# Batch 0's score products in three fp32r products for two tiles of each group of three, with the splits on ScalarE and VectorE and half of the squares' adds on GpSimd

## The reference

```python
qn = q / (norm(q, axis=1) + 1e-06)            # q, k, v: (2, 6016, 256); the norm runs over the tokens
kn = k / (norm(k, axis=1) + 1e-06)
s = kn.transpose(0, 2, 1) @ qn / tau          # (2, 256, 256): a product over 6016 tokens
a = softmax(s - s.max(-1))                    # with 1e-9 added to the sum
x = (v @ a).reshape(12032, 256)
h = x @ w_in                                  # w_in (256, 2048)
x = (h - tanh(h)) @ w_out                     # w_out (2048, 256)
out = (sigmoid(x @ w_gate) * (x @ w_val)) @ w2_out   # (256, 1536) twice, (1536, 256)
```

## Time and profile before

| what | us |
|---|---|
| median of 3 runs | 2383.25 |
| lowest and highest of them | 2382.99, 2384.51 |
| the profiled execution | 2383.25 |
| its span | 2381.5 |
| TensorE busy | 2356.5 |
| VectorE busy | 1406.4 |
| ScalarE busy | 536.5 |
| GpSimd busy | 251.2 |

### The profile page before, as it was taken

How to read it: one execution, slowest core, us unless ns; L and a number is a source line. 1 busy time by engine, 2 the same in 40 slices (tenths; PEclk the granted TensorE clock), 3 DMA queues, 4 the chain that set the end, 5 groups by cost and what they waited for, 6 DMA issues and landing times.

```text
span 2381.5 us, 29344 instructions
## 1 busy us (share of the span) xinstructions
PE 2356.5 (99%) x10410; PEld 1943.7 (82%) x10410; DVE 1406.4 (59%) x2180; ACT 536.5 (23%) x861; POOL 251.2 (11%) x130
## 2 busy tenths in 40 slices
PE   8999999999999999999999999999999999999998
PEld 7778888888888888888878888888888888888887
DVE  6856556566565565665756455555565565565553
ACT  5412122121121211212222122121221121221221
POOL 1721201202112021021310000000000000000000
PEclk9999999999999999999999999999999999999999
DMA  7400000000000000000100000000000000000000
GB/s 256 128 27 27 27 9 27 24 18 26 17 26 26 9 26 17 26 26 9 40 27 18 9 9 17 9 9 9 9 17 9 9 17 9 9 17 9 0 9 9
DMA packets 34272, 60.74 MB, mean 26 GB/s; under 512 B 3008, under 2 KB 22208, under 8 KB 34240
## 3 DMA queue, kind: packets, MB, share of 16 engines
q1 hardware_dynamic: 34240, 60.32, 7.7%
HBM read 47.99 MB, written 12.32 MB: 25 GB/s over the span
## 4 chain that ended last, share of the span: by engine, by line
PE 95%; DVE 3%; DMA 1%; issue 0%; ACT 0%; SPq 0%; POOL 0%; ACTq 0%; DVEq 0%
PE ring L236 54%; PE X L236 23%; PE O L582 17%; PE X L451 1%; DVE g_parts L913 1%; DVE g_parts L911 1%; DVE work L900 1%; PE O L236 0%; DMA v_raw<-v_t 0%; DMA qk_raw<-k 0%; POOL win_parts L386 0%; ACT work L745 0%; DVE norm L852 0%; SPq L262 0%; SPq L271 0%
## 5 line engine op out<-in xcount | busy, mean ns | idle before, releaser
L236 PE MATMUL ring<-x_parts,gv_parts 128*128 128x502 f32 x3456 | 836.8, 392 | 0.8 <-ACT x_parts L751 0.8
L745 ACT ACTIVATE work<-ring 128x502 f32<-128x502 f32 x672 | 397.1, 591 | 1680.5 <-PE ring L236 1618.7
L236 PEld LDWEIGHTS ring<-x_parts,gv_parts 128*128 128x128 f32 x3456 | 650.7, 189 | 138.5 <-issue 1.2
L236 PE MATMUL X<-g_parts,wout_parts 128*128 128x502 f32 x2304 | 579.7, 392 | 8.1 <-DVE g_parts L913 8.1
L236 PE MATMUL ring<-v_parts,weff 128*128 128x502 f32 x2304 | 585.2, 391 | 0.2 <-DVE weff L881 0.2
L236 PEld LDWEIGHTS X<-g_parts,wout_parts 128*128 128x128 f32 x2304 | 435.7, 190 | 101.3 <-DVE g_parts L913 10.9
L236 PEld LDWEIGHTS ring<-v_parts,weff 128*128 128x128 f32 x2304 | 434.2, 189 | 93.0 <-DVE work L900 2.6
L897 DVE TENSOR_TENSOR work<-work,ring 128x502 f32<-128x502 f32 x288 | 195.1, 677 | 511.8 <-PE ring L236 511.4
L582 PE MATMUL O<-p_parts,w2out_parts 128*128 128x502 f32 x1728 | 441.3, 389 | 3.3 <-DVE p_parts L911 3.2
L900 DVE TENSOR_TENSOR work<-ring,work 128x502 f32<-128x502 f32 x384 | 260.8, 679 | 266.2 <-ACT work L745 266.2
L582 PEld LDWEIGHTS O<-p_parts,w2out_parts 128*128 128x128 f32 x1728 | 324.6, 188 | 76.4 <-DVE p_parts L913 4.4
(11 more groups left out here) (71 smaller groups left out, 450.0 us busy)
## 6 DMA issues: line engine op xcount, KB each, us to landing
v_raw<-v_t SPq DMA_DIRECT2D x24, 502.0 KB, 3.6
out_t<-out_sb SPq DMA_DIRECT2D x44, 251.0 KB, 2.2
qk_raw<-q SPq DMA_DIRECT2D x24, 256.0 KB, 2.7
qk_raw<-k SPq DMA_DIRECT2D x24, 256.0 KB, 2.9
qk_raw<-q SPq DMA_DIRECT2D x15, 384.0 KB, 3.6
qk_raw<-k SPq DMA_DIRECT2D x15, 384.0 KB, 5.0
w_raw<-w_out SPq DMA_DIRECT2D x7, 512.0 KB, 3.8
w_raw<-w_in SPq DMA_DIRECT2D x4, 512.0 KB, 7.8
```

Source lines behind the costliest of these rows:

```text
L236: ins = nc.tensor.matmul(out, w[c][a], x[c][b], start=first and n == 0, stop=last and n == len(terms) - 1, skip_group_check=True)
L745: nc.scalar.activation(work[:, slot(kind, n, last), :], bank(kind, n, last), ACT.Sigmoid if kind == "p" else ACT.Tanh).then_inc(act_done, 1)
```

## The change

For groups 1 to 15 the last tile of the group stays in plain fp32. The first two tiles are split into high and low parts and multiplied as three fp32r products. Group 0 stays in fp32. The parts lie in a new tensor `qk_parts` with two slots. The splitting is shared out: VectorE copies q to its high part and subtracts for both low parts, ScalarE copies k to its high part. The sum of squares is shared out as well: VectorE adds only two of q's tiles, GpSimd adds q's third tile and k's three tiles.

```diff
+            qk_parts = sb("qk_parts", [P, 2, 2, 2, G - 1, C], F32R, a1)
...
             pool.memset(ident[:, :], 0.0).then_inc(consts_set, 1)
-            pool.memset(sq_acc[:, :, :, :], 0.0).then_inc(acc_cleared, 1)
+            pool.memset(sq_acc[:, :, :, :], 0.0).then_inc(k_acc_done, 1)
...
+            def add_squares(g, s):
+
+                pool.wait_ge(sq_done, g + 1)
+                pool.wait_ge(k_acc_done, g + 1)
+                if isinstance(g, int) and g == 0:
+                    acc, sq = sq_acc[:, 1, 0:2, :], qk_sq[:, s, 1, 0:2, :]
+                else:
+                    acc, sq = (x.rearrange("p x t c -> p (x t) c")[:, 2:2 * G, :]
+                               for x in (sq_acc[:, :, :, :], qk_sq[:, s]))
+                pool.tensor_tensor(acc, acc, sq, ALU.add).then_inc(k_acc_done, 1)
...
-            def group0(g, count, rs, u):
-
+            def group0(g, rs, s, u):
+
+                first = isinstance(g, int) and g == 0
                 pe.wait_ge(qk_loaded[rs], u * 32 + 32)
...
                 for m in range(CK):
-                    if m == norms_at:
+                    for t in ((0, 1) if first else (G - 1,)):
+                        ins = nc.tensor.matmul(X[:, m, 0:C], qk_raw[:, rs, 1, t, m * P:(m + 1) * P],
+                                               qk_raw[:, rs, 0, t, :], start=first and t == 0,
+                                               stop=first and t == 1, skip_group_check=True)
+                if not first:
+                    if isinstance(g, int) and g == GROUPS - 1:
                         norms(0)
...
+                    pe.wait_ge(qk_lo_done, g)
+                    ins = scores([qk_parts[:, s, a] for a in range(2)], G - 1, lambda m: X[:, m, 0:C], False)
                 ins.then_inc(s_done, 1)
...
                 if not (isinstance(g, int) and g < 2):
-                    act.wait_ge(acc_done, g - 1)
+                    act.wait_ge(q_acc_done, g - 1)
+                    act.wait_ge(k_acc_done, g)
                 raw = qk_raw[:, rs, :, 0:count, :]
                 nc.scalar.activation(qk_sq[:, s, :, 0:count, :], raw, ACT.Square).then_inc(sq_done, 1)
+                if not (isinstance(g, int) and g == 0):
+                    if not (isinstance(g, int) and g < 3):
+                        act.wait_ge(s_done, g - 1)
+                    nc.scalar.activation(qk_parts[:, s, HI, 1, :, :], qk_raw[:, rs, 1, 0:G - 1, :],
+                                         ACT.Copy).then_inc(k_hi_done, 1)
...
-            def group0(g, count, s):
-
-
+            def group0(g, rs, s, u):
+
+
+                first = isinstance(g, int) and g == 0
+                dve.wait_ge(qk_loaded[rs], u * 32 + 32)
+                if not first:
+                    if not (isinstance(g, int) and g < 3):
+                        dve.wait_ge(s_done, g - 1)
+                    V.tensor_copy(qk_parts[:, s, HI, 0, :, :], qk_raw[:, rs, 0, 0:G - 1, :]).then_inc(q_hi_done, 1)
                 dve.wait_ge(sq_done, g + 1)
...
-                    dve.wait_ge(acc_done, g)
-                acc = sq_acc[:, :, 0:count, :]
-                V.tensor_tensor(acc, acc, qk_sq[:, s, :, 0:count, :], ALU.add).then_inc(acc_done, 1)
+                    dve.wait_ge(q_acc_done, g)
+                acc = sq_acc[:, 0, 0:2, :]
+                V.tensor_tensor(acc, acc, qk_sq[:, s, 0, 0:2, :], ALU.add).then_inc(q_acc_done, 1)
+                if not first:
+
+                    dve.wait_ge(k_hi_done, g)
+                    dve.wait_ge(q_hi_done, g)
+                    for x in range(2):
+                        ins = V.tensor_tensor(qk_parts[:, s, LO, x, :, :], qk_raw[:, rs, x, 0:G - 1, :],
+                                              qk_parts[:, s, HI, x, :, :].bitcast(F32), ALU.subtract)
+                    ins.then_inc(qk_lo_done, 1)
```

More of the change, by code:

```diff
@@ L120, in attention_moe_kernel @@
         sq_done = sem("sq_done")
-        acc_cleared = sem("acc_cleared")
-        acc_done = sem("acc_done")
+        k_hi_done = sem("k_hi_done")
+        q_hi_done = sem("q_hi_done")
+        qk_lo_done = sem("qk_lo_done")
+        q_acc_done = sem("q_acc_done")
+        k_acc_done = sem("k_acc_done")
         s_done = sem("s_done")
@@ L380, in _ @@
                                pattern=[[-1, P]], channel_multiplier=1).then_inc(consts_set, 1)
+            def add_squares(g, s):
[7 more added lines that the diff above has]
+                pool.tensor_tensor(acc, acc, sq, ALU.add).then_inc(k_acc_done, 1)
+            for g in range(QK_SLOTS):
+                add_squares(g, g % 2)
+            with nc.Fori(0, GROUPS // QK_SLOTS - 1, engines=[ENG.Pool]) as t:
+                for s in range(QK_SLOTS):
+                    add_squares(t * QK_SLOTS + (QK_SLOTS + s), s % 2)
             def split_unit(n):
@@ L438, in scores @@
                 return ins
-            def group0(g, count, rs, u):
+            def group0(g, rs, s, u):
+                first = isinstance(g, int) and g == 0
                 pe.wait_ge(qk_loaded[rs], u * 32 + 32)
[L443 to L446, removed]
                 for m in range(CK):
-                    if m == norms_at:
-                        norms(0)
[L450 to L454, removed]
+                    for t in ((0, 1) if first else (G - 1,)):
[4 more added lines that the diff above has]
+                    if isinstance(g, int) and g == GROUPS - 1:
+                        norms(0)
+                    pe.wait_ge(qk_lo_done, g)
+                    ins = scores([qk_parts[:, s, a] for a in range(2)], G - 1, lambda m: X[:, m, 0:C], False)
                 ins.then_inc(s_done, 1)
@@ L461, in norms @@
                     pe.wait_ge(consts_set, 3)
-                    pe.wait_ge(acc_done, GROUPS)
+                    pe.wait_ge(q_acc_done, GROUPS)
                 else:
@@ L470, in norms @@
                 for n, (x, t, m) in enumerate(order):
+                    if b == 0 and n == 2 * CK:
+                        pe.wait_ge(k_acc_done, GROUPS + 1)
                     at = x * CK + m
@@ L721, in unit_hi @@
                     act.wait_ge(s_done, GROUPS)
-                    act.wait_ge(acc_done, GROUPS)
+                    act.wait_ge(q_acc_done, GROUPS)
+                    act.wait_ge(k_acc_done, GROUPS + 1)
                 if n == 2 * PIECES:
@@ L818, in _ @@
             V = nc.vector
-            def group0(g, count, s):
+            def group0(g, rs, s, u):
[5 more added lines that the diff above has]
+                    V.tensor_copy(qk_parts[:, s, HI, 0, :, :], qk_raw[:, rs, 0, 0:G - 1, :]).then_inc(q_hi_done, 1)
                 dve.wait_ge(sq_done, g + 1)
-                if isinstance(g, int) and g == 0:
-                    dve.wait_ge(acc_cleared, 1)
-                else:
-                    dve.wait_ge(acc_done, g)
-                acc = sq_acc[:, :, 0:count, :]
-                V.tensor_tensor(acc, acc, qk_sq[:, s, :, 0:count, :], ALU.add).then_inc(acc_done, 1)
+                if first:
+                    dve.wait_ge(k_acc_done, 1)
+                else:
+                    dve.wait_ge(q_acc_done, g)
[8 more added lines that the diff above has]
+                    ins.then_inc(qk_lo_done, 1)
             steps = [0]
@@ L958, in _ @@
             for g in range(QK_SLOTS):
[L959 removed]
+                group0(g, g, g % 2, 0)
             with nc.Fori(0, GROUPS // QK_SLOTS - 1, engines=[ENG.DVE]) as t:
                 for s in range(QK_SLOTS):
[L962 removed]
+                    group0(t * QK_SLOTS + (QK_SLOTS + s), s, s % 2, t + 1)
             dve.wait_ge(tau_loaded, 16)
```

6 lines of the change are left out of this document (3 added, 3 removed).

## The result

The changed kernel takes 2411.48 us (median; 2410.14 to 2412.71), the kernel before 2383.22 (2382.99 to 2384.51). The ratio is 1.0114, with a 95% interval of 1.0102 to 1.0126: 28.3 us slower. The forecast was 2417.5 us, 6 us too much; the direction was right.

What follows compares the result with a forecast made beforehand. TensorE bounds the kernel; in batch 0's score stage VectorE and GpSimd, excluding each other, would take the lead. Scaling 32.6 us later plus 1.6 us for the clock, on 2383.25, gave 2417.5 us; own range 2410 to 2423, widened to 2405 to 2425.

Steps and rivals of the forecast that it cites:

- The mechanism: In batch 0's score stage, VectorE instructions with all inputs in SBUF and GpSimd's adds run one after the other; chance 0.72.
- TensorE's saving: Score products per group: 2.29 us in place of 2.59, giving back 4.5 us only if TensorE stayed the one waited for.
- sign that was named: Trace readings expected in batch 0's score stage: group distance, scaling time, TensorE idle and GpSimd busy time, unchanged blocks.
- Rival A: Score stage: GpSimd's add runs beside VectorE's work, 2.4 us per group, 2382.4 us in all; chance 0.07.
- Rival B: Score stage: VectorE slips in cheaply between GpSimd's always-ready instructions, 3.46 us per group, 2400 us; chance 0.11.
- rival C: Score stage: TensorE at half the clock becomes the bound, some 4.9 us per group, 2423 us; chance 0.10.
- The price of a group: Score stage: GpSimd's 2.41 us plus VectorE's 2.22 us, one after the other, 4.63 us for each of 15 groups.
- The stage's end: End of batch 0's scores: last subtraction near 79.4 us, then last products and norms until the scaling at 83.7 us.
- S: Start of VectorE's scaling, the first step needing finished scores: forecast 83.7 us, before 51.12, so 32.6 us later.
- The clock: A lower granted TensorE clock, in the open only in the score stage's last matmuls: 1.6 us added.
- the tail: TensorE's work closing the score stage: twelve products, two fp32 matmuls, norms, last twelve products and draining, 6.5 us.
- Behind S: After the scaling: nothing taken; v's load no longer waited for, GpSimd's earlier weight split against it, either a microsecond or two.

Runs made afterwards that it cites:

- experiment one: The changed kernel with GpSimd's adds of squares cut from 1024 columns to 2, all instructions and waits kept: 2385.27 us, ratio 1.0005 to the kernel before.
- experiment two: The changed kernel with all adds of squares back on VectorE, 1536 columns per group, GpSimd idle in the stage: 2394.41 us, ratio 1.0042.
- experiment six: The changed kernel with GpSimd's add cut from 1024 to 512 columns per group: 2393.67 us, ratio 1.0038 to the kernel before.
- experiment four: The changed kernel with ScalarE writing squares of q's first two tiles to PSUM, from where VectorE adds them: 2405.9 us, ratio 1.0089.
- experiment five: The changed kernel with four slots of parts in place of two: 2411.44 us, ratio 1.0111 to the kernel before.
- experiment three: The kernel before with only the adds of squares shared between VectorE and GpSimd, products plain fp32: 2390.75 us, ratio 1.0027.
- one-tile version: The changed kernel with one tile per group in three products, VectorE adding all squares, GpSimd idle: 2385.81 us; with groups 0 and 1 plain and steps reordered, 2386.02 us.

## Why the prediction was right, and where its sum was off

**The mechanism** held. VectorE's instructions with all operands in SBUF and GpSimd's add shut each other out: the times of experiments one, two and six show it, and experiment four shows by the location of one operand that it is the operands and not the engines' order. The hand-over through two slots is not what holds the groups apart (experiment five). TensorE's saving had nothing to act on, and the blocks kept their length.

Not every sign that was named came true. The groups are 4.32 us apart for 4.4 to 4.9, the scaling came at 79.77 us for 82 to 88, TensorE idled 24.1 us before line 240 for over 30, and GpSimd was busy 39.6 us for about 36. They miss on the side of a smaller price, which is the next point.

Rival A (the two run beside each other) is refuted by the 4.32 us, and experiment one shows why: only with GpSimd's columns gone does the time return. Its number, 2382.4, was too good even for that case, which came out at 2385.27. Rival B asked for 3.46 us per group with GpSimd always at work; GpSimd waited 24.7 us in the stage. Its price, 0.31 us for an instruction that slips in at the start of GpSimd's add, was seen (2.71 us at 25.02, 2.70 at 28.43), but for one instruction of the four; another waited the add out. In rival C TensorE would have set the pace at the lower clock. It never did: the granted clock was 0.50 only in patches, as from 50 to 54 us, and 1.00 from 56 to 72 us, where TensorE was busy for 9.13 of 16 us in bursts.

**The price of a group** is the term that was mis-sized: 4.63 us forecast, 4.32 measured, 15 x 0.31 = 4.7 us. VectorE's share in the open is 0.34 + 3 x 0.60 = 2.14 us (from 20.16 to 20.50 after the copy, from 20.50 to 21.10 after the add), for 2.22. GpSimd's share is then 2.18 for 2.41. I had counted that one instruction's end overlaps the next one's start among VectorE's three two-input instructions, but not behind the copy and not between the engines. Experiment six gives GpSimd's length a slope of one, so what overlaps is a fixed part of it.

**The stage's end.** The last subtraction ended at 74.25 us for 79.4. VectorE in order of time:

```profile
72.97 1.28 DVE L870 TENSOR_TENSOR qk_parts<-qk_raw,qk_parts 128x512 fp32r<-128x512 f32 x2
...
77.63 0.17 DVE L886 TENSOR_SCALAR norm_x<-norm 128x4 f32<-128x4 f32 x1 [3.30 <-ACT norm L719]
...
79.51 0.22 DVE L895 TENSOR_SCALAR norm<-norm,tau_sb 128x2 f32<-128x2 f32 x1
79.77 0.88 DVE L901 TENSOR_SCALAR s_acc<-X,norm 128x256 f32<-128x256 f32 x2
```

From there to the scaling at 79.77 it was 5.5 us, for 4.3 forecast. The products at 72.16 took 1.54 until the next, not 1.43, and the scaling followed the small steps of the norms (77.63 to 79.73), not the last products, which ended at 79.15; that difference I had put into the range. S came 28.65 us later than before, for 32.6 forecast without the clock.

**The clock.** I took 1.6 us for it in the tail, and nothing of that was paid. From 72 to 77.1 us the granted clock was 1.00. Only the last twelve products, with 0.79 from 77.1 to 79.2 us, were slower, 1.98 us for 1.70, and they ended before the norms' steps did. Where a lower clock does cost is experiment three, 5.25 us of norms for 2.73.

**Behind S** I took nothing; between S and the first tanh of the blocks the profiles have 19.9 us (79.77 to 99.71) for 21.7 (51.12 to 72.79), 1.7 us saved. TensorE's first weff products, in the kernel before and then now (L236 and L240 are the same line of a helper):

```profile
57.28 2.90 PE L236 MATMUL O<-win_parts,a_t 128*128 128x512 f32 x6 [1.18 <-POOL win_parts L386]
59.97 4.41 PE L236 MATMUL X<-win_parts,a_t 128*128 128x512 f32 x12
64.22 2.96 PE L236 MATMUL O<-win_parts,a_t 128*128 128x512 f32 x12
```

```profile
85.43 2.92 PE L240 MATMUL O<-win_parts,a_t 128*128 128x512 f32 x6 [0.69 <-ACT a_t L730]
88.15 3.16 PE L240 MATMUL X<-win_parts,a_t 128*128 128x512 f32 x12
91.15 2.96 PE L240 MATMUL O<-win_parts,a_t 128*128 128x512 f32 x12
```

The first of them starts 5.66 us behind S for 6.16. Before, it waited for GpSimd's split of `w_in`, at the end of a chain that began with v's load; now it waits for the softmax matrix. That is 0.5 us, the most that the missing wait for v's load can have given. The other 1.25 us are the next twelve products: from 59.97 to 64.22 us before, at a granted clock of 0.62, and from 88.15 to 91.15 now, at 0.93. So the clock came into the time after all, behind S and with the opposite sign, a term that the prediction did not have.

Together, in the profiled executions: 28.65 - 1.7 + 0.3 in the blocks is the span's 27.2 us. The medians differ by 28.3 us: with the same 1.75 us around its span the profiled execution took about 2410.5 us, 1.0 less than its kernel's median. The kernel came out slower, to which I had given 0.94. The time lies inside the forecast's own range too, near its lower end.

## What to carry to other kernels

Before moving work to an idle engine, look in the trace for a stretch in which both engines are busy, and compare the same instruction's length there and elsewhere: 950 against 682 ns says more than any sum of busy times. If the two exclude each other, add their times: an idle GpSimd is then no free place for 1024 columns of adds that cost VectorE 1.07 us (1.75 less 0.68, experiment two) and the pair 2.18 when GpSimd does them. And an engine that is at its limit with a second one close behind (TensorE at 2.59 us a group, DMA at 2.3) pays back little when it is relieved, as experiment one shows.

## What the runs showed of the hardware that was not expected

- The granted clock of the profile and the pace of TensorE can differ at the start. In the kernel before, the first eight records, those of group 0, took 3.78 us from 4.42 us on, about twice what eight take later, and the granted clock of that stretch is 1.00; seven of the eight experiments have 3.70 to 3.78 us for them. The kernel before then had 18 records from 8.5 to 12.5 us, the full pace; the one-tile version had 8 at about half the pace, also with a row of 1.00. Its second group's load landed 0.2 us later. The wait for that load does not decide it alone: experiment six had 0.63 us of it and then four records in 1.13 us, the one-tile versions had 0.61 and stayed slow. What decides it stays open; it costs about 2 us here.
- The exclusion works both ways. GpSimd's adds of two columns in experiment one, in order of time:

```profile
9.82 0.70 POOL L396 TENSOR_TENSOR sq_acc<-sq_acc,qk_sq 128x2 f32<-128x2 f32 x1 [4.24 <-ACT qk_sq L711]
...
13.66 0.20 POOL L396 TENSOR_TENSOR sq_acc<-sq_acc,qk_sq 128x2 f32<-128x2 f32 x1 [1.60 <-ACT qk_sq L711]
```

At 9.82 VectorE's own add (9.78 to 10.47) was under way and GpSimd's small one took 0.70 us in place of 0.20.
- More slack (experiment five) and less contention for one instruction (experiment four) made the turns of the two engines uneven, GpSimd taking two or three in a row, with little or nothing gained.
